# A fused attention and two-layer expert kernel: RMS norm's inverse root computed on four token columns and spread through DRAM, and one gate block moved ahead of a tile's last down block

## The reference

```python
# 1: linear attention with decay, step by step over t
y[:, :, t] = einsum('bhd,bhde->bhe', r_t, state + (u * k_t) outer v_t)
state = w * state + k_t outer v_t
# 2: x = y as 3072 x 384 tokens
g = x @ w_gate;  x = (g * sigmoid(g) * (x @ w_val)) @ w_out          # 384 -> 1536 -> 384
# 3: the same with a norm in front
rms = sqrt(mean(x * x, axis=-1) + 1e-6);  xn = x / rms * rms_g
g = xn @ w2_gate;  out = (g * sigmoid(g) * (xn @ w2_val)) @ w2_out
```

## Time and profile before

| | us |
|---|---|
| the three runs | 998.73, 1001.45, 1001.85 |
| their median | 1001.45 |
| the profiled execution's own time | 1003.28 |
| span of the profile, first to last instruction | 1001.4 |
| PE busy | 962.8 (96%) |
| DVE busy | 703.7 (70%) |
| POOL busy | 565.2 (56%) |
| ACT busy | 401.7 (40%) |
| mean granted TensorE clock | 0.995 of full |

### The profile page before, as it was taken

The page is one execution under the profiler, slowest core; times in us unless marked ns, Lnnn a source line. Parts: engine busy times, 40 slices in busy tenths (PEclk is TensorE's granted clock), DMA queues, the critical chain, the costliest instruction groups (busy, mean ns, idle before and its releaser), DMA issues.

```text
span 1001.4 us, 23699 instructions
## 1 busy us (share of the span) xinstructions
PE 962.8 (96%) x9324; PEld 798.7 (80%) x9324; DVE 703.7 (70%) x1123; ACT 401.7 (40%) x839; POOL 565.2 (56%) x446
## 2 busy tenths in 40 slices
PE   4898999999999999999999999999999999999998
PEld 4898997888888888888878777777888777878876
DVE  7896767666757767675528968788777889577760
ACT  3362334334433433433342364433543436444423
POOL 8797977564666665565242234778527688211134
PEclk9998999999999999999999999999999999999999
DMA  6663443425354442533141146434054441254201
GB/s 254 217 214 106 126 165 115 148 99 187 138 174 141 159 148 98 169 142 116 74 161 62 64 179 222 158 112 151 32 201 157 158 151 60 89 185 158 79 0 63
DMA packets 50348, 136.06 MB, mean 136 GB/s; under 512 B 6656, under 2 KB 9664, under 8 KB 50240
## 3 DMA queue, kind: packets, MB, share of 16 engines
q1 hardware_dynamic: 50240, 134.56, 38.7%
HBM read 108.29 MB, written 25.17 MB: 133 GB/s over the span
## 4 chain that ended last, share of the span: by engine, by line
PE 73%; POOL 9%; DVE 8%; issue 6%; DMA 2%; ACT 1%; SPq 0%; POOLq 0%; DVEq 0%; ACTq 0%
PE ps_down L808 7%; PE ps_down L810 6%; PE ps_down L809 6%; PE ps_val L808 5%; PE ps_val L810 5%; PE ps_val L809 5%; PE ps_gate L808 5%; PE ps_gate L810 5%; PE ps_gate L809 5%; PE ps_level L901 4%; PE ps_level L1054 2%; PE ps_level L1056 2%; PE ps_level L1055 2%; PE ps_val L954 1%; PE ps_val L1054 1%
## 5 line engine op out<-in xcount | busy, mean ns | idle before, releaser
L1821 POOL TENSOR_TENSOR h_lo<-h_raw,h_hi 128x512 fp32r<-128x512 f32 (+1 forms) x84 | 114.9, 1368 | 209.1 <-ACT h_hi L1156 200.3
L808 PE MATMUL ps_down<-h_hi,down_hi 128*128 128x512 f32 (+1 forms) x360 | 135.5, 376 | 3.5 <-POOL h_lo L1821 2.4
L810 PE MATMUL ps_down<-h_lo,down_hi 128*128 128x512 f32 (+1 forms) x360 | 133.0, 369 | 0.0
L809 PE MATMUL ps_down<-h_hi,down_lo 128*128 128x512 f32 (+1 forms) x360 | 133.0, 369 | 0.0
L1422 DVE TENSOR_TENSOR h_raw<-h_raw,ps_val 128x512 f32<-128x512 f32 (+1 forms) x84 | 51.1, 608 | 86.6 <-PE ps_val L810 79.2
L1156 ACT ACTIVATE h_hi<-h_raw 128x512 fp32r<-128x512 f32 (+1 forms) x84 | 47.9, 571 | 154.6 <-DVE h_raw L1422 154.5
L808 PE MATMUL ps_gate<-x_hi,up_weights 128*128 128x512 f32 (+1 forms) x252 | 94.4, 375 | 1.3 <-ACT h_raw L1150 1.3
L808 PE MATMUL ps_val<-x_hi,up_weights 128*128 128x512 f32 (+1 forms) x249 | 91.1, 366 | 2.8 <-DVE h_raw L1422 2.7
L810 PE MATMUL ps_gate<-x_lo,up_weights 128*128 128x512 f32 (+1 forms) x252 | 91.4, 363 | 1.5 <-issue 1.5
L809 PE MATMUL ps_gate<-x_hi,up_weights 128*128 128x512 f32 (+1 forms) x252 | 91.3, 362 | 0.0
L1864 POOL TENSOR_TENSOR pair_prod<-chunk_in,w_block 128x768 f32<-128x768 f32 x47 | 91.2, 1942 | 0.0
(11 more groups left out here) (293 smaller groups left out, 2461.0 us busy)
## 6 DMA issues: line engine op xcount, KB each, us to landing
ring<-sums_dram SPq DMA_DIRECT2D x72, 640.0 KB, 4.8
r_block<-in_r_blk_dram SPq DMA_DIRECT2D x24, 768.0 KB, 4.9
chunk_in<-in_a_t_dram SPq DMA_DIRECT2D x24, 512.0 KB, 3.7
chunk_in<-in_a_n_dram SPq DMA_DIRECT2D x24, 384.0 KB, 4.5
sums_dram<-sum_lo SPq DMA_DIRECT2D x24, 320.0 KB, 2.9
staging<-in_weights_dram SPq DMA_DIRECT2D x18, 384.0 KB, 4.1
raw<-in_blocks_dram SPq DMA_DIRECT2D x8, 576.0 KB, 5.8
sums_dram<-sum_hi SPq DMA_DIRECT2D x12, 320.0 KB, 2.4
```

Source lines behind the costliest of these rows:

```text
L808: nc.tensor.matmul(dst, w_hi, x_h, start=first, stop=False)
L809: nc.tensor.matmul(dst, w_lo, x_h, start=False, stop=False)
L810: return nc.tensor.matmul(dst, w_hi, x_l, start=False, stop=last)
L1821: nc.gpsimd.tensor_tensor(h_lo[:, f % 3, 0:WIDTH[t]], h_raw[:, f % 2, 0:WIDTH[t]], h_hi[:, f % 3, 0:WIDTH[t]].bitcast(F32), ALU.subtract). ...
```

## The change

Two things are changed.

1. **The inverse root.** The sum of squares is the same in all 128 rows. ACT now copies one row of it out of PSUM (`copy_row`, 1x512), SP moves that row by DMA into 128 partitions of four columns (`turn_sums`), DVE does all 15 operations of the inverse root on 128x4 (`invert`), for all six tiles, each operation waiting for the one before, and SP stores the 512 results to DRAM and reads them back into all 128 rows (`spread_inverse`). POOL's and DVE's Newton steps on 128x512 are gone. PE, which took its bank back when DVE had read the sums, now does so when ACT has. In the last tile of stage 1 the norms and the sums stand at other slots.
2. **The gate block.** In the first two tiles (256 tokens each) PE does gate 0 of the next tile ahead of down 11 of this one, and no longer at the next tile's slot 0.

```diff
-NORM_AT = (6, 7)
-SUM_AT = [21 + i * 6 // len(SUMMED) for i in range(len(SUMMED))]
-MADE_AT = [22 + i * 13 // NPROD for i in range(NPROD)]
+NORM_AT = (8, 9)
+INVERSE_AT = (12, 12)
+NORM_X_AT = (16, 17)
+SUM_AT = [18 + i * 9 // len(SUMMED) for i in range(len(SUMMED))]
+MADE_AT = [19 + i * 16 // NPROD for i in range(NPROD)]
+ROW_STEP = ((1, 8), (2, 17))
+TURN_AT = (7, 15)
+INVERSE_STEP = ((1, 16), (2, 25))
+SPREAD_AT = (9, 17)
+AHEAD = 2
...
+            def turn_sums(k):
+                sp.wait_ge(row_copied, k + 1)
+                sp.dma_start(turned(k)[:, 0, :], norm_of(k)[1][0:1, :].rearrange("o (p j) -> o p j", j=TOK // P))\
+                  .then_inc(turned_in[k % 2], 16)
+
+            def spread_inverse(k):
+                sp.wait_ge(inverse_done, k + 1)
+                sp.dma_start(inverse_dram[k].rearrange("(p j) -> p j", j=TOK // P), turned(k)[:, 1, :]).then_inc(inverse_stored, 16)
+                sp.wait_ge(inverse_stored, 16 * (k + 1))
+                sp.dma_start(norm_of(k)[0], inverse_dram[k].unsqueeze(0).broadcast_to([P, TOK])).then_inc(inverse_in[k % 2], 16)
...
+                    for n in range(2):
+                        if r + 1 < ROUNDS and g % GROUPS == TURN_AT[n]:
+                            turn_sums(2 * r + 2 + n)
+                        if r + 1 < ROUNDS and g % GROUPS == SPREAD_AT[n]:
+                            spread_inverse(2 * r + 2 + n)
...
-                                pe.wait_ge(norm_step, (2 * r + 2 + q - 2) * 3 + 1)
+                                pe.wait_ge(row_copied, 2 * r + 2 + q - 2 + 1)
...
-                    group(t, kind, f)
+                    if t < AHEAD and s == SLOTS - 1:
+                        group(t + 1, "gate", 0)
+                    if not 0 < t <= AHEAD or s > 0:
+                        group(t, kind, f)
...
+            def copy_row(k):
+                place = bank[6 + k] if k < 2 else bank[BANKS[k // 2 - 1][1 + k % 2][4]]
+                act.wait_ge(norm_summed, k + 1)
+                nc.scalar.activation(norm_of(k)[1][0:1, :], place[0:1, :], ACT.Copy).then_inc(row_copied, 1)
...
+                dve.wait_ge(turned_in[k % 2], 16 * (k // 2 + 1))
+                chain(nc.vector.tensor_scalar(half, half, 0.5 / DM, 0.5e-6, ALU.mult, ALU.add))
+                chain(nc.vector.tensor_scalar(y.bitcast(I32), half.bitcast(I32), 1, None, ALU.logical_shift_right))
+                chain(nc.vector.tensor_scalar(y.bitcast(I32), y.bitcast(I32), -1.0, float(0x5F3759DF - 0x400000), ALU.mult, ALU.add))
+                for i in range(3):
+                    chain(nc.vector.tensor_tensor(z, y, y, ALU.mult))
+                    chain(nc.vector.tensor_tensor(z, z, half, ALU.mult))
+                    chain(nc.vector.tensor_scalar(z, z, -1.0, 1.5, ALU.mult, ALU.add))
+                    last = nc.vector.tensor_tensor(y, y, z, ALU.mult)
...
-                if k < 2:
-                    dve.wait_ge(newton_dve, 12 * (k + 1))
-                else:
-                    dve.wait_ge(newton, 12 * (k - 1))
+                dve.wait_ge(inverse_in[k % 2], 16 * (k // 2 + 1))
...
-                            for i in range(3):
-                                newton_step(2 * r + 2 + n, i, 0)
-                                newton_step(2 * r + 2 + n, i, 1)
```

More of the change, by code:

```diff
@@ L592, in build @@
         norm_step = sem("norm_step")
+        row_copied = sem("row_copied")
+        turned_in = [sem(f"turned_in{i}") for i in range(2)]
+        inverse_done = sem("inverse_done")
+        inverse_stored = sem("inverse_stored")
+        inverse_in = [sem(f"inverse_in{i}") for i in range(2)]
         down2_lo_dve = sem("down2_lo_dve")
@@ L780, in _ @@
                 load_ring(g)
+                if g == 0:
+                    for k in range(2):
+                        turn_sums(k)
+                    for k in range(2):
+                        spread_inverse(k)
                 if g < PAIRS - 2:
@@ L1579, in sum_end @@
                     nc.vector.tensor_tensor(after, after, sums_out(g, 1), ALU.add).then_inc(state_done, 1)
-            def norm(k):
-                def chain(ins, n):
-                    ins.then_inc(norm_step, 1)
[L1585 to L1603, removed]
-                else:
-                    dve.wait_ge(newton_dve, n)
-                    nc.vector.tensor_tensor(b, one_half[:, :].broadcast_to([P, TOK]), b, ALU.subtract).then_inc(newton_dve, 1)
-                    dve.wait_ge(newton_dve, n + 1)
-                    nc.vector.tensor_tensor(a, a, b, ALU.mult).then_inc(newton_dve, 1)
+            def invert(k):
+                half, y, z = turned(k)[:, 0, :], turned(k)[:, 1, :], turned(k)[:, 2, :]
+                done = [14 * k]
+                def chain(ins):
+                    done[0] += 1
+                    ins.then_inc(norm_step, 1)
+                    dve.wait_ge(norm_step, done[0])
+                dve.wait_ge(turned_in[k % 2], 16 * (k // 2 + 1))
[7 more added lines that the diff above has]
+                    last = nc.vector.tensor_tensor(y, y, z, ALU.mult)
+                    if i < 2:
+                        chain(last)
+                last.then_inc(inverse_done, 1)
@@ L1775, in _ @@
                         for k in range(2):
-                            if s == NORM_AT[k] + 1:
-                                norm(k)
-                            for i in range(3):
-                                for part in range(2):
-                                    if s == NORM_AT[0] + 2 + 6 * k + 2 * i + part:
-                                        newton_step(k, i, part)
-                            if s == NORM_AT[0] + 8 + 6 * k:
+                            if s == INVERSE_AT[k]:
+                                invert(k)
+                            if s == NORM_X_AT[k]:
                                 norm_x(k)
@@ L1802, in _ @@
                         for n in range(2):
-                            if r + 1 < ROUNDS and NORM_STEP[n] == (q, s - 1):
-                                norm(2 * r + 2 + n)
+                            if r + 1 < ROUNDS and INVERSE_STEP[n] == (q, s):
+                                invert(2 * r + 2 + n)
                             if r + 1 < ROUNDS and NORM_X[n] == (q, s):
@@ L1878, in add_squares @@
             def add_squares(k, kt):
-                a, b, half = norm_of(k)
+                a, b = norm_of(k)
                 pool.wait_ge(squared[k % 2], KT * (k // 2) + kt + 1)
@@ L1996, in _ @@
                         add_squares(2 * r + 2, 2)
-                    for n in range(2):
-                        if r + 1 < ROUNDS and NORM_STEP[n][0] == q:
-                            for i in range(3):
-                                newton_step(2 * r + 2 + n, i, 0)
-                                newton_step(2 * r + 2 + n, i, 1)
                 for p in SUMMED[SUMS_BEFORE[0]:SUMS_BEFORE[1]] if r + 1 < ROUNDS else ():
@@ L2092 @@
     sums = nc.dram_tensor("sums_dram", (GROUPS, 2, P, GROUP), F32, kind="Internal").ap()
-    build(nc, *args, out, x2, sums)
+    inverse = nc.dram_tensor("inverse_dram", (TILES2, TOK), F32, kind="Internal").ap()
+    build(nc, *args, out, x2, sums, inverse)
     got = run_bass_kernel_spmd(nc, [arrays], core_ids=[0]).results[0]["out_dram"]
```

39 lines of the change are left out of this document (13 added, 26 removed).

## The result

The changed kernel takes 1002.08 us (median of 22 runs, 1000.0 to 1004.44), the kernel before 999.14 (median of 22 runs in the same comparison). The ratio is 1.0022, 95% interval 1.0013 to 1.0031: slower by 0.22%, some 2 us, where 4.6 us less was forecast. The ratio is that of the means of all executions; the two medians are 2.9 us apart. The time lies inside the stated range of 991 to 1003.5, but on the other side of the kernel before.

What follows compares the result with a forecast made beforehand. The prediction took TensorE (PE) as the bound nearly everywhere, with only its gaps and low-clock stretches to win. Terms −4.1 − 1.0 − 3.8 + 5.3 − 1.0 = −4.6 us gave a median of 996.9 us, range 991 to 1003.5.

Steps and rivals of the forecast that it cites:

- C: Last tile of stage 1: four PE waits for a gate/val product should go, −3.8 us (−3.8 to 0).
- D: Rounds 0 and 1: inverse chain of D = 2.9 us on DVE delays PE at steps 21 and 28, 4D − 6.26 = +5.3 us.
- E: Pass 3 of rounds 0 and 1: relieved POOL and DVE let norm_x come sooner, −1.0 us (0 to −6.8).
- A: Tile 0 to 1: gate 0 fills PE's 2.45 us wait and the clock stays up, −4.1 us (other end −1.05).
- B: Tile 1 to 2: gate 0 fills PE's 1.43 us wait for a_mat, −1.0 us (0 to −1.4).
- rival 3: Pass 3: broadcast late behind the 640 KB load, landing at 679.5, term +4 instead of −1.0, 1001.9 us; chance 0.12.
- The rival drawn from that page: Rounds 0 and 1: inverse chain an estimated 2.4 us without gaps, term +3.3 instead of +5.3; no chance given.
- At nothing: Parts priced at zero: ACT's six row copies, POOL's relief, held-back ring loads; the turned row is on its way eight steps ahead.
- its own case: The main forecast for the whole kernel, −4.6 us to 996.9, own range 993.5 to 1000.5; chance 0.53.

Runs made afterwards that it cites:

- norm only: The changed kernel with the gate blocks back in their old places (AHEAD = 0): 1003.61 us, ratio 1.0035 to the kernel before.
- last tile only: The kernel before with the small inverse root and new slots only in stage 1's last tile, gate blocks in old places: 994.85 us, ratio 0.9953.
- before again: The kernel before, unchanged, run once more for the granted clock of each execution: 998.96 us, ratio 0.9995.

## Why the prediction was wrong

The terms, predicted and measured. The last column is from the ratios above: C is the last tile alone, D the gain with one Newton step, E what is left of the 9.4 after D. A and B can't be told apart by ratios (together they gave 2.5 alone, 1.3 with the new norm everywhere, 2.5 with it in the last tile only); there B is from the undisturbed profiles, and A is the estimate of 0.8 us from the 40 executions.

| term | predicted | between the two profiles | by ratios |
|---|---|---|---|
| A, gate block at tile 1 | −4.1 | −4.3 | −0.8 (estimate; no fall: 0) |
| B, gate block at tile 2 | −1.0 | −1.1 | −1.1 |
| C, last tile | −3.8 | −5.0 | −4.7 |
| D, chains in rounds 0 and 1 | +5.3 | +5.0 | +5.5 |
| E, pass 3 | −1.0 | +4.0 | +3.9 |

The terms of the middle column add to −1.4; with 1.1 us that an unexplained wait of PE at 141.63 ("issue") was shorter in the profile after (it is 0.33 to 1.45 in the twelve profiles), and 0.4 the other way in small pieces, they come to the −2.06 of the profiles. Those of the last column add to +2.8, where +2.2 was measured.

*Step A: right in its mechanism, wrong as a price.* Val 0 started at 94.71, where 94.9 was forecast, and gate 1 at 95.85, where 96.2 was; the full clock came. But the 4.1 us were the price of a clock fall that most executions of before do not have, and without it the edit gives nothing there. The three times of before already said so: 998.73 beside 1001.45 and 1001.85, and a profiled execution at 1003.28 with a mean clock of 0.995. The prediction took the 1.83 us between the profile and the median off as a constant, when that excess was a part of the very fall that it then counted as a gain.

*Step E: the step that decided the sign.* The prediction had: "with 8 KB in 2.8 us twice, the result lands at about 675.5, before 673.95 + 2.7 = 676.6". The store took 4.2 us and the broadcast 4.8 (in the profile after, from issue to landing), 9.0 instead of 5.6. The broadcast moves 256 KB and not 8, so its nearest row was the ring load's 4.8 and not the small DMA's 2.8. In the prediction's frame, with the 11.36 us put back that were won ahead of round 0, the result landed at 679.1. PE pays for it with a wait of 1.83 us in round 0 and of 1.15 in round 1, and in round 0 with 1.6 us of lower clock. That was rival 3, which had the landing (679.5) and the term (+4 for E) right, at a chance of only 0.12; with A at its typical price the two together give the measured sign. What comes free in pass 3 was there all the same, and perhaps more than the 1.0 us forecast: with one Newton step and the broadcast in time the kernel is 3.0 us faster by the ratios (0.9898 against 0.9928, give or take 2.8) than with the old norms in rounds 0 and 1.

*Step D: right.* 2.87 us against 2.9 for the chain, and 1.14 and 1.38 us of shift against 1.2 and 1.5. The chain's slope and its room are confirmed by one and by five Newton steps. The Trainium skill, "VectorE: DVE Perf Modes", section "⚠️ The TRN2 errata — SBUF-src ops pay a fixed extra latency per instruction", has a fixed 151 cycles in an fp32 tensor_tensor, an estimated 0.16 us at four columns; the trace agrees with 0.16. The six tensor_scalar of the fifteen, of which that figure does not speak, took 0.16 to 0.17. The rival drawn from that page, a chain of 2.4 us without gaps and +3.3 for D, did not come: the operations start 0.2 us apart, and the 60 of them cost PE about 5 us.

*Step C: right, and a little small.* A wait costs more than its idle time. Rows of PE around one in the undisturbed profile of before:

```profile
561.69 0.39 PE L810 MATMUL ps_gate<-x_lo,up_weights 128*128 128x512 f32 x1
562.55 0.50 PE L808 MATMUL ps_val<-x_hi,up_weights 128*128 128x512 f32 x1 [0.48 <-DVE h_raw L1422]
562.89 0.39 PE L809 MATMUL ps_val<-x_hi,up_weights 128*128 128x512 f32 x1
```

From start to start it is 0.86 and 0.34 where two steps of 0.23 stand otherwise: 0.74 us lost for a wait shown as 0.48. Four waits of 3.80 us together with 0.26 each are 4.84, near the 4.7 and 5.0 measured.

*At nothing:* right. POOL's 59 us less, ACT's row copies, the turned rows (DVE never waits for one) and the ring loads held back: no PE wait names them.

*Slips in its sums* that moved nothing: D = 4.0 gives 4D − 6.26 = 9.7, not 9.9. The upper end of its own case, with D at 3.4, half of C missing and E gone, is 1001.8 and not 1000.5. And seven slots of the ring are seven of the 24 groups of a round of 134 us, 39 us of PE's work and not 20.

The Trainium skill's "DMA: Bandwidth & Descriptors", section "Anatomy of one DMA — SWDGE (gpsimd) path", gives DMAs on GpSimd's path about 2 us fixed and 436 KB per us beside it, by which the store and the broadcast would be an estimated 4.6 us. Here SP issues them, and the trace has 9.0. No fixed time describes it: the same store of 2 KB took 4.2 us when it was issued right behind a 640 KB load, 2.2 one place earlier in the queue, and 1.8 in the kernel with its Newton steps on POOL.

## What to carry to other kernels

Before a stretch of low clock in a profile is counted as something to win, ask how many executions have it: compare the profiled execution's own time and mean clock with the other runs, take a second profile, and price the edit at both levels. When a value goes through a store and a load in one in-order DMA queue, follow each instruction in that queue: what it waits for, what large transfer it stands behind, and its own bytes; here one place in the queue was worth 6.9 us, more than the 5.5 us that the arithmetic of the inverse root cost PE in rounds 0 and 1. And a chain of tiny dependent operations belongs on an engine that is idle, or where nothing is queued behind it that the bound engine waits for: here the same chain moved to POOL gave back 3.5 of the 5.5 us.

## What was not expected of the hardware

The same wait of PE (2.2 to 2.5 us at 90 us) is followed by a fall of the clock to the lower level in some executions and not in others. Behind 2.45 us the granted clock was 0.50 for some 10 us, behind 2.42 (norm only) for some 7; behind 2.43 (last tile only) and 2.18 (before again) it stayed 1.00. The length of the wait does not decide it: a wait of 1.42 us at the start of tile 2 was followed by a fall in the profile with the norm only and by none in that of the last tile only, and with five Newton steps the clock fell behind 2.72, 2.53 and 2.73 us and not behind 2.54. What decides it is open.

PE's first steps behind a wait take longer too. Behind five waits measured like the one under step C, of 0.48 to 1.83 us, PE lost 0.24 to 0.27 us more than the idle time shown, in stage 1 and in stage 2 alike.
